# A chunked delta-rule attention with two expert layers: the first pair's short products in another order and in two parts, the second pair's blocks transposed by TensorE

## What is computed

```python
k_n = k / (np.linalg.norm(k, axis=-1, keepdims=True) + 1e-06)
for t in range(S):
    y[:, :, t] = np.einsum('bhd,bhde->bhe', q[:, :, t], state)
    v_old = np.einsum('bhde,bhd->bhe', state, kt)
    state = state + bt[:, :, :, None] * np.einsum('bhd,bhe->bhde', kt, vt - v_old)
...
h = np.maximum(np.maximum(x @ w1, x @ w2), x @ w3); x = h @ w_out
# then a top-2 gate over 8 experts, each relu(x @ w1[e]) @ w2[e], weighted and added
```

## Time and profile before

| | us |
|---|---|
| median of 3 runs | 1025.61 |
| lowest, highest | 1025.16, 1026.86 |
| the profiled execution, its own time | 1025.56 |
| its span, first to last instruction | 1023.8 |
| TensorE busy | 997.9 (97%) |
| VectorE busy | 721.6 (70%) |
| ScalarE busy | 469.7 (46%) |
| GpSimd busy | 214.8 (21%) |
| first product of the loop (L1895) starts at | 67.46 |

### The profile page before, as it was taken

How to read it: one execution, slowest core, us unless ns; L and a number is a source line. 1 busy time by engine, 2 the same in 40 slices (tenths; PEclk the granted TensorE clock), 3 DMA queues, 4 the chain that set the end, 5 groups by cost and what they waited for, 6 DMA issues and landing times.

```text
span 1023.8 us, 25726 instructions
## 1 busy us (share of the span) xinstructions
PE 997.9 (97%) x10425; PEld 929.1 (91%) x10425; DVE 721.6 (70%) x1701; ACT 469.7 (46%) x700; POOL 214.8 (21%) x229
## 2 busy tenths in 40 slices
PE   8899999999999999999999999999999999999995
PEld 7888898898888888888899999999999999999995
DVE  7988795893884786543569677778677686776772
ACT  4542345226325325233363546546465465654651
POOL 0464310210120130121315221212211112212111
PEclk8899999999999999999999999999999999999998
DMA  9540320420430330116656625234352526526221
GB/s 306 129 109 2 94 53 23 129 61 3 126 85 3 78 93 2 57 42 217 220 188 179 186 43 169 47 88 122 53 156 47 170 39 172 163 55 169 40 30 24
DMA packets 71190, 101.68 MB, mean 99 GB/s; under 512 B 28608, under 2 KB 59584, under 8 KB 70720
## 3 DMA queue, kind: packets, MB, share of 16 engines
q1 hardware_dynamic: 59024, 78.10, 25.4%
q0 software_dynamic: 10992, 20.70, 10.5%
q10 hardware_dynamic: 1088, 1.65, 0.5%
HBM read 136.98 MB, written 29.51 MB: 163 GB/s over the span
## 4 chain that ended last, share of the span: by engine, by line
PE 92%; DVE 3%; ACT 3%; issue 2%; POOLq 0%; POOL 0%; ACTq 0%; DVEq 0%
PE ps L1895 43%; PE ps L2061 20%; PE ps L1944 8%; PE ps L1744 3%; PE ps L2072 3%; PE ps L1874 2%; PE ps L1850 2%; PE ps L1725 2%; PE ps L1862 2%; PE ps L1960 2%; PE ps L1784 1%; DVE prod L1176 1%; DVE x L1180 1%; PE ps L1830 1%; ACT solve L862 1%
## 5 line engine op out<-in xcount | busy, mean ns | idle before, releaser
L1895 PE MATMUL ps<-xr,wr_in 128*128 128x512 f32 x972 | 235.8, 396 | 0.3 <-ACT xr L888 0.3
L1895 PEld LDWEIGHTS ps<-xr,wr_in 128*128 128x128 f32 x972 | 178.6, 188 | 39.6 <-DVE wr_in L1298 0.5
L1895 PE MATMUL ps<-xbT,w1r 128*128 128x256 f32 x1728 | 211.6, 283 | 0.6
L1895 PEld LDWEIGHTS ps<-xbT,w1r 128*128 128x128 f32 x1728 | 209.7, 192 | 2.5 <-issue 2.1
L2061 PE MATMUL ps<-w2r,hbT 128*128 128x384 f32 x1152 | 205.9, 336 | 0.0
L2061 PEld LDWEIGHTS ps<-w2r,hbT 128*128 128x128 f32 x1152 | 198.9, 188 | 0.0
L754 POOL DMA_INDIRECT out_rows<-yb,idx x55 | 91.5, 1664 | 374.8 <-DVE yb L1524 289.1
L965 ACT ACTIVATE hbT<-ps 128x512 fp32r<-128x512 f32 x96 | 57.3, 597 | 166.6 <-PE ps L1895 163.4
L1336 DVE TENSOR_TENSOR w1r<-w1s,w1r 128x768 fp32r<-128x768 f32 x124 | 117.3, 956 | 17.2 <-ACT w1r L949 15.1
L949 ACT CAST w1r<-w1s 128x768 fp32r<-128x768 f32 x124 | 101.2, 828 | 24.8 <-DMA w1s<-in_we 24.8
L1336 DVE TENSOR_TENSOR w2r<-w2s,w2r 128x768 fp32r<-128x768 f32 x124 | 110.2, 950 | 2.0 <-ACT w2r L953 2.0
(11 more groups left out here) (232 smaller groups left out, 1125.6 us busy)
## 6 DMA issues: line engine op xcount, KB each, us to landing
w1s<-in_we SPq DMA_DIRECT2D x31, 1536.0 KB
w2s<-in_we SPq DMA_DIRECT2D x31, 1536.0 KB
xb<-rows SPq DMA_DIRECT2D x24, 402.0 KB
kv_s<-in_kv SPq DMA_DIRECT2D x24, 384.0 KB, 3.7
k_s<-in_k SPq DMA_DIRECT2D x12, 512.0 KB, 4.0
joint<-in_q SPq DMA_DIRECT2D x24, 256.0 KB
out_rows<-padrow SPq DMA_DIRECT2D x13, 384.0 KB, 4.3
w_in<-in_w_blocks SPq DMA_DIRECT2D x3, 1152.0 KB, 9.7
```

What stands on the lines that cost most here:

```text
L1895: mm = pe.matmul(dst, w, m, start=(opens and n == 0), stop=(closes and n == len(todo) - 1))
```

## The change

The second pair's diagonal blocks are no longer transposed by VectorE (`rows_of(1)` goes) but by 128 TensorE matmuls of 32x32 against the identity, behind `first_k_q`, with a filler of 512 columns after each 32 of them; ScalarE copies them from PSUM into the rows, which lie in `diag` itself (`row_blocks`). The opening 8 fillers become 2 of 512 columns, the 32 fillers of base steps 18 to 30 become 4 at step 30, and all later ones go. Both low products stand ahead of the first corner. The outputs of chunk 0 are made in two halves (one by PSUM bank of each half of the partitions), the second one behind `k_state_and_q(1)` and in H_BANKS. u of chunk 1 and its outputs are made and copied in halves; its outputs stand ahead of its state step, half of which stands ahead of the transposes of y and half behind; that step uses C_BANKS, so gram(5) waits for the state. GpSimd does its weight splits later and 15 base steps instead of 12. The queues of ScalarE and VectorE are rearranged to fit.

```diff
-        POOL_STEPS = {1: 12, 2: 11}
+        POOL_STEPS = {1: 15, 2: 11}
...
             if t == 0 and n == 1:
-                return early + (Q - 1 - early) * min(i + 1, low) // low
+                return early + (Q - 1 - early) * min(max(i - 2, 0), low - 3) // (low - 3)
...
@@ GpSimd
             first_pT(0)
-            weights_low(0)
             zero_x(1)
             pool.wait_ge(s_xz, 2)
             first_pT(1)
             pool.wait_ge(p_low, 1)
             pool.wait_ge(s_off, 4)
             nc.gpsimd.tensor_copy(off[:], off_early).then_inc(s_off_moved, 1)
+            weights_low(0)
             pool_base(1)
...
@@ ScalarE
+            def blocks_in_rows():
+
+                act.wait_ge(p_rows, 1)
+                nc.scalar.copy(row_blocks[1][:].rearrange("p (k i) b -> p k (i b)", k=2), ps[:, E_BANKS:E_BANKS + 2]
+                               ).then_inc(s_gb, 1)
...
-            weights_high(0, 4)
+            folded_gate()
+            weights_high(0, 2)
             first_k_q()
-            folded_gate()
+            blocks_in_rows()
+            roots(1)
+            weights_high(2, 4)
             first_low(0)
             first_solve(0, 0)
             first_solve(0, 1)
             first_corner(0)
-            roots(1)
             first_low(1)
             first_solve(1, 0)
             first_solve(1, 1)
             u_out(0)
             first_corner(1)
             first_state()
-            y_out(0)
+            first_y_half(0)
             out_weights_high()
-            u_out(1)
+            first_y_half(1)
+            first_u_half()
+            second_u_half()
+            second_y_half(0)
+            second_y_half(1)
+            x_high(0)
             weights_high(4, FT)
-            y_out(1)
-            x_high(0)
...
@@ VectorE
-            rows_of(1)
+            norms(1, (0, 1))
             first_corner_half(0)
-            norms(1, (0,))
-            u_half(0)
+            norms(1, (2,))
+            first_u()
             first_corner_half(1)
-            norms(1, (1,))
             first_state()
-            norms(1, (2,))
             scaled_v(1)
-            weights_low(1, (0, 1))
+            weights_low(1, (0,))
             r_out(1)
-            pT_out(1, (0,))
-            weights_low(1, (2,))
-            u_half(1)
-            pT_out(1, (1,))
+            pT_out(1)
+            second_u_half()
+            weights_low(1, (1, 2))
+            second_y_half(0)
+            second_y_half(1)
             norm_columns(1)
+            weights_low(2, (0,))
+            x_low(0)
+            weights_low(2, (1, 2))
             state_out(1)
-            y_half(1)
-            weights_low(2)
-            x_low(0)
...
@@ TensorE
+            def keep_warm_wide(bank):
+
+                pe.matmul(ps[:, bank].rearrange("p (a b) -> p a b", b=P), ones[:], bc(ones[:], 4), start=True, stop=True)
...
+            def blocks_to_rows():
+
+                pe.wait_ge(s_diag, 4)
+                pe.wait_ge(s_const, N_CONST)
+                for i in range(Q):
+                    for g in range(4):
+                        rows = slice(g * Q, g * Q + Q)
+                        mm = pe.matmul(ps[rows, E_BANKS + i // (Q // 2), i % (Q // 2) * Q:(i % (Q // 2) + 1) * Q],
+                                       diag[rows, :, i], ident[rows, rows], start=True, stop=True)
+                    if i == Q - 1:
+                        mm.then_inc(p_rows, 1)
+                    if i % 8 == 7:
+                        keep_warm_wide(C_BANKS)
...
+            def second_outputs(n):
+
+                if n == 0:
+                    pe.wait_ge(s_u_half, 2)
+                    pe.wait_ge(s_pT, 3)
+                else:
+                    pe.wait_ge(s_u, 4)
+                outputs_of(1, n, D_BANKS).then_inc(p_y if n else p_y_half, 1)
...
-            for n in range(8):
-                pe.matmul(ps[:, C_BANKS + n % 4, n // 4 * P:n // 4 * P + P], ones[:], ones[:], start=True, stop=True)
+            keep_warm_wide(C_BANKS)
+            keep_warm_wide(C_BANKS + 1)
...
             first_k_q()
-            for k in range(18, Q - 2):
-                keep_warm(E_BANKS + 1, 2, k)
-            keep_warm(E_BANKS + 1, 8, Q - 2)
+            blocks_to_rows()
+            keep_warm(C_BANKS, 4, Q - 2)
             first_low(0)
-            keep_warm(C_BANKS, 3)
+            first_low(1)
             first_corner(0)
-            first_low(1)
             solve_u(0)
             first_corner(1)
             state_step(0)
-            outputs(0)
+            first_outputs(0)
             k_state_and_q(1)
-            keep_warm(H_BANKS, 3)
+            first_outputs(1)
             solve_u(1)
-            keep_warm(H_BANKS, 3)
-            state_step(1)
-            outputs(1)
+            second_outputs(0)
+            second_outputs(1)
+            state_step(1, (0,))
             pe.wait_ge(s_const, N_CONST)
-            keep_warm(C_BANKS, 4)
             to_xT(0, 0)
             to_xT(0, 1)
-            keep_warm(C_BANKS, 4)
+            state_step(1, (1,))
```

132 lines of the change are left out of this document (91 added, 41 removed).

## The result

| | before | after |
|---|---|---|
| median of 22 runs each, us | 1025.09 | 1026.68 |
| lowest, highest | 1023.99, 1029.35 | 1025.92, 1027.84 |
| profiled execution: own time, span | 1025.56, 1023.8 | 1026.15, 1024.4 |
| first product of the loop starts at | 67.46 | 68.51 |
| second pair's k times state starts at | 86.19 | 87.08 |

The account below looks back on a forecast made before the run. The bound was taken to be the chain of short TensorE steps and copies between them ahead of the first product, 38.86 to 67.46 us. Gains of 2.2 and 2.5 us gave 1025.56 - 4.76 = 1020.8 us, range 1019.4 to 1025.0.

Parts of the forecast that it names:

- The halves: 2.2 and 2.5 us: Outputs of the first chunk in halves gain 2.2 us; halves and new order in the second chunk gain 2.5 us.
- 23.8 of the sum: Predicted time from the low products at 38.86 to the first product at 62.7: 23.8 us.
- Worth nothing by themselves: Fillers removed behind the low product all stood in waits, so removing them was priced at nothing.
- rival E: Clock stays at 1.2 GHz through the chain without fillers behind 38.86: 1038.7 us, slower than before; chance 0.06.
- Norms: "nothing gained or lost": Second pair's norms take 1.92 us in place of VectorE's 1.93 us transpose; u starts at 43.55 against 43.61.
- The rows: ready at 35.7, cost nothing: Second pair's TensorE transposes give rows at 35.7, covered by VectorE's base steps, with 0.5 us to spare.
- the one instruction stop: The late instruction block stops the first state step by about 0.9 us; the 0.69 and 1.05 us stops go.
- rival C: Strided weight reads make the transposes take 8.8 instead of 4.4 us, so rows come late: 1024.7 us; chance 0.12.
- The clock from 29.5 on: Gap-free new transposes raise the granted clock near 29.5 instead of 32.87; it stays at 1.0 from there.
- Rival B: Clock drops at the chain's end, round transposes without fillers; first products start at the low level: 1022.5 us; chance 0.14.
- Rival D: Second pair's margin, shrunk from 1.7 to 0.3 us, goes negative if GpSimd needs 2 us more: 1022.5 us; chance 0.08.
- the forecast's 62.7: Predicted start of the loop's first product, 62.7 instead of 67.46 us.

Follow-up runs that it names:

- h0: g1 with wide 512-column fillers, two ahead of the low products and one on either side of the first corner, for its short ones; 0.9987 of the kernel before.
- i0: h1 with the whole of the second piece's norms on VectorE behind the first state copy; 0.9993 of the kernel before.
- f4: The changed kernel with the edits of f2 and f3 together: GpSimd wait, ten fillers, rows ahead of their fillers; 1.0012 of the kernel before.
- h2: h1 with 14 instead of 15 GpSimd base steps for the second pair, and the steps asked for one block earlier; 0.9995 of the kernel before.
- h1: h0 with VectorE forming first_u ahead of the second piece's norms and ScalarE copying the low product ahead of weight splits; 1.0003 of the kernel before.
- g3: The kernel before without its 17 fillers behind the low product, nothing else changed; 1.002 of the kernel before, median 1021.79 against 1019.72 us.
- f1: The changed kernel with one more wait: GpSimd's masking product and all behind it wait for VectorE's second-pair norms; 1.0002 of the kernel before.
- g4: The changed kernel with eight fillers instead of four at base step 30; 1.0015 of the kernel before.
- f3: The changed kernel without wide fillers among the transposing products; 128-column fillers behind them, two per base step 22 to 29, eight at 30; 1.0033 of the kernel before.
- g1: f1 with eight fillers instead of four at base step 30 and three on either side of the first corner; 0.9999 of the kernel before.
- e4: The changed kernel with VectorE transposing the second pair's blocks again, and the old fillers, norms and roots places; 1.0007 of the kernel before.
- g2: Only the halves and new order; VectorE's transposes, norms, GpSimd work and early fillers as before, three fillers either side of the first corner; 1.0005 of the kernel before.
- e2: The changed kernel with the first chunk's corner copy ahead of the last three norm operations in VectorE's queue; 0.9999 of the kernel before.
- e1: The changed kernel with six 128-column fillers between the first corner product and the first u; 1.001 of the kernel before.
- f2: f1 with ten fillers: three behind the low products, four behind the first corner, three behind the second; 0.9992 of the kernel before.

## Why the prediction was wrong, by its own steps

- *The halves: 2.2 and 2.5 us.* Right: 2.0 and 2.35. From the end of the first state step to the product 13.85 us were measured for 13.3 predicted, 18.2 before; u, outputs, half a state and transposes follow one another with waits of 0.34, 0.31 and 0.25. From the low products on, clean executions need 24.0 and 24.2 us (h0, i0) for the 23.8 of the sum. But these start 3 to 6 us late (44.80, 41.84), so that VectorE's norms lay ahead of the chain; so do the other two under 25.1 us, f4 and h2. Where the low products of the new order started by 39.6, it took 25.6 to 33.1. The two parts were each reached (h1: 10.2 us from low products in time to the end of the state step; the change: 13.85 behind it), never both in one profile. And 1.05 of the first gain is a stop that the one profile of before happened to show.
- *"Worth nothing by themselves"*, the fillers removed. Wrong, and one of the two steps that decided it. I priced them as work in a wait and not as what keeps the clock. g3 measures 2.0 us in the kernel before. In the change the low level lasts from 44.0 to 54.25; u, the second corner and the state step alone lose 3.2 us by it (3.65, 1.92 and 2.58 for 2.07, 1.20 and 1.64). This is rival E's mechanism, in a smaller size: the level came back by itself at 54.25. My argument against E was that the level held through the bursts before; six filler records stood among those bursts, and more behind them.
- *Norms: "nothing gained or lost".* Wrong, the other deciding step, and in time the first. I took them as long as the first pair's (1.92 us for all), which GpSimd does not disturb. They took 4.9 (41.02 to 45.88), and u waited 2.55 us; f1 shows the cause by removing it. The change had moved GpSimd's product from 44.82, where it disturbed nobody, to beside them. The kernel before shows the sign: L1136, the same operation as L1196, took 0.59 us (0.18 in h0 and i0, where nothing stood beside it) and ended (44.78) with GpSimd's memset (44.74), as VectorE's and GpSimd's timelines of before have it:

```profile
44.19 0.59 DVE L1136 TENSOR_SCALAR nrm<-nrm 128x32 f32<-128x32 f32 x1
```
```profile
43.80 0.94 POOL L690 MEMSET x<- 128x1024 f32 x1
44.82 2.34 POOL L673 TENSOR_TENSOR joint<-joint,after_row 64x1024 f32<-64x1024 f32 x1
```

  I had not asked what GpSimd does at the moments to which VectorE's work was moved. The Trainium skill, "SBUF — State Buffer", section "Who interferes with whom", states the rule: a VectorE instruction with two SBUF inputs contends with a GpSimd one that reads SBUF, and a form with two ports with any, for the whole instruction. The trace agrees in each case: beside the memset, which only writes, the two-input L1192 took 0.21, while the scalar L1196 took 0.51 and ended with it; beside the product the two-input L1201 took 2.03 and the reciprocal L1199 kept its 0.35.
- *The rows: ready at 35.7, cost nothing.* Wrong by 2.7 us (38.44). I put the one instruction stop into the state step; it fell in the transposes (1.20 us here, up to 2.90 in h0). My own count of blocks has borders there too, every 128 records, and I had looked at it only behind 38.86. The rest is the three fillers between them, 1.99, 1.38 and 2.00 us for the 0.9 that I took. And ScalarE has weight splits behind its copy, so the low copy came at 42.27 for 40.12. That is rival C's place, but not its cause: the transposes took about the 4.4 us of the sum, not 8.8. By the rule that I had cited from the Trainium skill, "SBUF — State Buffer", Door 1, they should have been slower; no run shows that. In the change this delay was hidden behind the norms: in g4 the low products came 0.9 us earlier and u started no sooner.
- *The clock from 29.5 on.* Wrong: it rose at 30.4, fell again at 33.8 behind the stop, and rose at 37.2.
- *Rival B*, the clock at the end of the chain: it did not come in the changed kernel, where the level was high from 54.25 to the product; the transposes of y took 1.50 us, the length at the full clock, there and in all its edits. It did come in f3, for 1.6 us, behind a stop of 1.75; g1 had a stop of 1.87 at the same place and kept the level, so what brought it stays open. The rule that I had cited from the Trainium skill, "TensorE: Matmul & The Clock Gate", Part 4, that transposes don't count, did not decide here: the level that cost the change its time fell ahead of u.
- *Rival D*, the second pair's margin: not in the change, whose product came late (27.13 us to L1871, no wait), but in e4, g2 and i0, where GpSimd's or VectorE's base steps start later or the product earlier: 1.4 to 1.8 us. Had the forecast's 62.7 come, part of it would probably have gone here; my 0.3 us of margin was the warning.

The front lost 5.4 us and the halves won 4.3: 1.05 at the product, 0.9 at the second pair's k times state, 0.6 between the two profiled times, 1.6 between the medians. In this profile 3.04 of the 5.4 lie before u, on the chain of the norms, and 2.34 behind it, at the low level (3.2 us by the clock, less a stop of 0.69 that before had there). What each cause is worth over many executions can't be added up from single edits: each wait removed uncovers the next (e2, h1) or moves the fall of the clock (e1). Open also: why the level falls at other moments in each execution; and a version with the chain clean, rows in time and base steps in time was not found, h0_wide at 0.9987 being the nearest. The forecast's 4.8 us was reached by none.

## What to carry to other kernels

Before pricing a filler at nothing, take it out alone and read the granted clock; and when work is moved on VectorE, look what GpSimd does at the new place, operation by operation, for here operations with two inputs or with a scalar lasted until GpSimd's ended (0.19 us became 2.03, 0.18 became 0.51). A chain shortened by several edits needs its front as exact as its end: here a late front ate the whole gain. And judge such a change by many runs, since one profile can show either level of the clock.

## What the runs showed of the hardware that was not expected

- TensorE busy for 17.07 us on end at the low level (f2), while in h0 and f4 nearly the same work ran for 27 and 28 us at the high level. In these three traces the level that had been gained was kept, and the one that was lost was not gained anew by such products.
- The 32-column transposes took the same time at both levels: 64 records 1.13 us at a granted clock of 0.50 (27.52 and 34.34 in the change) and 1.11 at 1.00 (37.33). The corner product, 32 columns too, took 1.92 for 1.20, and a filler of 512 columns 1.99 for 1.13.
- The supply of instructions: bursts of these transposes broke off after their 117th record or so (the 51st of the second group) in thirteen of the fourteen profiles that have them, and in f3, f4 and g1 again 128 records later. That distance, 128 products with as many weight loads, agrees with the block of 256 instructions that the prediction read from two stops. In f3 and f4 the second block came 3.7 and 3.5 us behind the first:
```profile
33.33 2.04 PE L1845 MATMUL ps<-ident,diag 32*32 32x32 f32 x128 [3.92 <-issue]
```
  How long the stop lasts differs, and it sorts the twelve profiles with fillers among the transposes: six have 1.20 to 2.90 us, and their low products start at 40.3 to 44.8; six have under 0.5, and theirs start at 38.4 to 39.6. The DMA share before it doesn't decide: 1.30 in the change, but 1.38 in f2, which hardly stopped.
- VectorE's and GpSimd's operations hold each other: in f1, the scaling of blocks took 2.61 us instead of 1.23 beside GpSimd's product, and GpSimd's copy 1.92 instead of 1.04.
